# A convolution and two feed-forward layers on one core: the first chunk's tap products are summed by TensorE, its load is split, and the first matmul group starts on parts of its input

## The chip, the cores and the metric

The kernel runs on one core of one Trainium2 chip. The metric is the device time of one execution in microseconds (us), the median of the runs; lower is better.

## The reference

`x` is [2, 4096, 192], `weight_gen` [2, 4096, 8, 7], `w_in` of both layers [192, 2048] and `w_out` [2048, 192], all float32. The reference computes

```
w = exp(wg - max(wg)); w = w / (sum(w) + 1e-9)                 # softmax over the 7 taps
y[b,s,h,g] = sum_k w[b,s,h,k] * x_pad[b, s+k, h, g]            # 6 zero tokens ahead of each sequence
h = y @ w_in1;  g = maximum(0.01*h, h);  y1 = g @ w_out1
h = y1 @ w_in2; r = maximum(h, 0);       out = (r*r) @ w_out2
```

Each of the 192 columns belongs to one of 8 heads of 24; a token's output is the sum of 7 products, each of a window that starts one token later than the last.

## The kernel before

**Chunks and segments.** Partition p holds 64 successive tokens. A chunk is 4 tokens of every partition (512 tokens), and there are 16 chunks. A segment is one layer on one chunk, 32 in all, in the order s = 0, 1 (layer 1 of chunks 0 and 1), then 2 (layer 2 of chunk 0), 3 (layer 1 of chunk 2), and so on in turn. Each float32 operand of a matmul is split into a high part (a copy rounded to fp32r) and a low part (the difference); three products high x high, high x low, low x high make one. The copies and high parts are made by ScalarE (`in_hi` L293, `out_hi` L299, `x_hi` L309 and L312), the low parts by VectorE (`in_lo` L429, `out_lo` L437 and L438, `x_lo` L497 to L502).

**Steps of a segment.** A segment has 8 up steps and 8 down steps. An up step (L700) is 18 matmuls of 512 columns, in 9 pairs, where the two of a pair use the upper and the lower 64 rows of the array, and it fills the two banks of an `h_pair`; there are two such pairs of banks, used in turn. ScalarE then makes `g_hi` (L352) and `g` (L356) of it, VectorE `g_lo` (L569); in layer 2, ScalarE makes `u` (L358), VectorE `g` (L560), ScalarE `g_hi` (L364) and VectorE `g_lo`. A down step (L719, L723) is 20 such matmuls. The order on TensorE is written out in `steps_of`: up 0, up 1, up 2, up 3, down 0, up 4, down 1, up 5, down 2, down 3, up 6, down 4, up 7, down 5, with downs 6 and 7 behind the next segment's ups 0 and 1. Up n waits until `g` of up n-2 has been made (`pair_free`); `g` of n waits for `g_lo` of n-2. In segments 0 and 2 the turn (below) stands between down 4 and up 7.

**The convolution of a chunk** is a list of 19 VectorE operations (`conv_ops`): 6 for the softmax (L450 to L468, with one exp on ScalarE, L303), 7 products of 128x768 (L479) and 6 additions (L484, the last in two halves, L487 and L490). The result is turned by 12 transposes (`turn_x`, L665 and L668) into the h_pair, and `x_hi`, `x_lo`, then `spread_hi` (L320 to L322) and `spread_lo` (L519 to L521) copy it so that each half of the partitions holds what its matmuls need. All of these end before up 0 starts: it waits for both spreads.

**Order of the start.** SP issues, in this order: tap logits of chunk 0 (L208), its window (L198 the 4 tokens of each partition, L203 twice for the 6 tokens of halo), `w_in` piece 0 (L223 and three of L227), `w_out` piece 0 (L237), `w_in` 1, logits and window of chunk 1, `w_out` 1, `w_in` 2, `w_out` 2, `w_in` 3. A layer's weights come in 4 pieces of each kind, in two buffers of each kind, so `w_in` q waits for `in_lo` q-2 and `w_out` q for `out_lo` q-2. VectorE makes chunk 0's convolution with `in_lo` 0, `out_lo` 0 and `in_lo` 1 between its operations, then `x_lo` and `spread_lo`, then two softmax operations of chunk 1. ScalarE makes exp 0, `in_hi` 0, `out_hi` 0, `in_hi` 1, `x_hi`, `spread_hi`. In segment 0 both engines have chunk 1's convolution and the further pieces between the steps (table `IN_FIRST`; pieces at j = 0, 2, 4, 6), in segments 1 and 2 chunk 2's (`IN_SECOND`, `IN_THIRD`) and the pieces of layer 2. Up j with even j in segments 0 and 2 waits for `in_lo` of its piece, and down j for `out_lo`. POOL zeroes the halo of the first rows and makes the identity.

```
conv_ops(0, range(SOFT + 4)); in_lo(0); conv_ops(0, range(SOFT + 4, SOFT + 7)); out_lo(0)
conv_ops(0, range(SOFT + 7, SOFT + 10)); in_lo(1); conv_ops(0, range(SOFT + 10, CONV))
x_lo(0, ...); spread_lo(0, 0); conv_ops(1, (0, 1))            # VectorE ahead of segment 0
```

## Time and profile before

| | us |
|---|---|
| median of 3 runs (lowest to highest) | 1191.36 (1190.73 to 1193.7) |
| the profiled execution | 1191.39 |
| its span, first to last instruction | 1189.6 |
| TensorE matmul busy | 1150.2 (97%) |
| weight loads busy | 1089.3 (92%) |
| VectorE / ScalarE busy | 862.7 (73%) / 668.7 (56%) |

The span leaves about 1.8 us of the profiled execution outside of it. Matmuls overlap in pairs, so the busy time of TensorE says that it is occupied, not that each matmul is as short as it can be; the start-to-start distance of a step says more.

### The profile page before, as it was taken

What the parts mean: (1) busy time and instruction counts of PE and PEld (TensorE: products, weight loads), DVE (VectorE), ACT (ScalarE), POOL (GpSimd) and SP (SyncE); (2) the same over time, 40 slices, a digit from 0 to 9 for tenths busy, and PEclk for the clock granted to TensorE, in tenths of its full rate; (3) what the DMA queues carried; (4) which work ended last, traced back from release to release, by engine and by line L of the source; (5) the groups of instructions that cost most, each with busy time, mean ns of one, the idle gap of its engine ahead of it and who ended that gap; (6) DMA issues with size and microseconds to landing.
All of it is one profiled execution on the core that took longest, in us unless ns stands there. A gap on an engine that the chain in (4) does not pass through costs nothing.

```text
span 1189.6 us, 22593 instructions
## 1 busy us (share of the span) xinstructions
PE 1150.2 (97%) x10112; PEld 1089.3 (92%) x10112; DVE 862.7 (73%) x1048; ACT 668.7 (56%) x817; POOL 3.8 (0%) x11
## 2 busy tenths in 40 slices
PE   0999999999999999999999999999999999999997
PEld 0789899999999999999999999999999999999996
DVE  6778687776778667687776878667687776874664
ACT  2675556646565555555646556565555555556553
POOL 1000000000000000000000000000000000000000
PEclk9999999999999999999999999999999999999999
DMA  8210101000010100101000010100101001000000
GB/s 203 68 54 1 38 15 38 14 27 12 14 38 15 38 1 15 39 15 38 7 17 30 14 38 15 38 1 15 38 14 38 1 15 39 14 1 15 1 1 27
DMA packets 15233, 31.58 MB, mean 27 GB/s; under 512 B 1572, under 2 KB 10914, under 8 KB 15136
## 3 DMA queue, kind: packets, MB, share of 16 engines
q1 hardware_dynamic: 15136, 30.14, 8.1%
q8 instruction: 79, 1.29, 0.5%
q14 instruction: 18, 0.15, 0.0%
HBM read 23.84 MB, written 6.29 MB: 25 GB/s over the span
## 4 chain that ended last, share of the span: by engine, by line
PE 94%; DVE 4%; ACT 1%; DMA 1%; issue 0%; SPq 0%; DVEq 0%; ACTq 0%
PE h_pair L700 44%; PE y_main_psum L719 29%; PE y_rest_psum L723 19%; DVE tap_product L479 1%; DVE conv_out L484 1%; DVE g_lo L569 1%; DMA x_window<-in_x_dram 1%; PE h_pair L665 0%; PE h_pair L679 0%; PE h_pair L682 0%; DVE w_in_parts L429 0%; PE h_pair L668 0%; DVE w_out_parts L438 0%; DVE conv_out L479 0%; DVE w_out_parts L437 0%
## 5 line engine op out<-in xcount | busy, mean ns | idle before, releaser
L700 PE MATMUL h_pair<-x_parts,w_in_parts 64*128 64x512 f32 x4608 | 616.1, 392 | 6.7 <-issue 5.5
L700 PEld LDWEIGHTS h_pair<-x_parts,w_in_parts 64*128 64x128 f32 x4608 | 537.7, 185 | 35.1 <-issue 6.9
L719 PE MATMUL y_main_psum<-g_hi,w_out_parts 64*128 64x512 f32 x2048 | 531.8, 394 | 0.1
L569 DVE TENSOR_TENSOR g_lo<-g,g_hi 128x1024 fp32r<-128x1024 f32 x256 | 313.2, 1223 | 149.7 <-ACT g_hi L364 87.3
L719 PEld LDWEIGHTS y_main_psum<-g_hi,w_out_parts 64*128 64x128 f32 x2048 | 343.6, 185 | 12.2 <-DVE g_lo L569 0.5
L723 PE MATMUL y_rest_psum<-g_lo,w_out_parts 64*128 64x512 f32 x1024 | 297.4, 391 | 0.0
L719 PE MATMUL y_main_psum<-g_lo,w_out_parts 64*128 64x512 f32 x1024 | 297.1, 391 | 0.0
L723 PE MATMUL y_rest_psum<-g_hi,w_out_parts 64*128 64x512 f32 x1024 | 296.7, 391 | 0.0
L352 ACT ACTIVATE g_hi<-h_pair 128x1024 fp32r<-128x1024 f32 x128 | 131.6, 1028 | 197.4 <-PE h_pair L700 197.3
L364 ACT ACTIVATE g_hi<-g 128x1024 fp32r<-128x1024 f32 x128 | 135.8, 1061 | 169.9 <-DVE g L560 169.9
L560 DVE SCALAR_TENSOR_TENSOR g<-h_pair,u 128x1024 f32<-128x1024 f32 x128 | 156.4, 1222 | 72.4 <-ACT u L358 71.7
L723 PEld LDWEIGHTS y_rest_psum<-g_lo,w_out_parts 64*128 64x128 f32 x1024 | 173.7, 185 | 6.1
L723 PEld LDWEIGHTS y_rest_psum<-g_hi,w_out_parts 64*128 64x128 f32 x1024 | 173.9, 185 | 5.5
L719 PEld LDWEIGHTS y_main_psum<-g_lo,w_out_parts 64*128 64x128 f32 x1024 | 173.6, 185 | 5.7
L358 ACT ACTIVATE u<-h_pair 128x1024 f32<-128x1024 f32 x128 | 130.6, 1020 | 79.9 <-PE h_pair L700 78.9
L356 ACT ACTIVATE g<-h_pair 128x1024 f32<-128x1024 f32 x128 | 130.8, 1022 | 1.5 <-DVE g_lo L569 1.5
L479 DVE TENSOR_TENSOR tap_product<-x_window,tap_weights 128x768 f32<-128x768 f32 x96 | 89.9, 952 | 0.0
L484 DVE TENSOR_TENSOR conv_out<-conv_out,tap_product 128x768 f32<-128x768 f32 x80 | 76.2, 953 | 0.5
L531 DVE TENSOR_TENSOR raw_w_in<-y_main_psum,x_window 128x512 f32<-128x512 f32 x16 | 11.1, 692 | 62.5 <-ACT x_window L333 62.5
L333 ACT ACTIVATE x_window<-y_main_psum 128x512 f32<-128x512 f32 x32 | 19.1, 597 | 30.6 <-PE y_rest_psum L723 30.6
L665 PE MATMUL h_pair<-identity,conv_out 64*128 64x64 f32 x128 | 9.8, 228 | 25.2 <-DVE conv_out L490 25.2
L665 PEld LDWEIGHTS h_pair<-identity,conv_out 64*128 64x128 f32 x128 | 9.5, 143 | 26.4 <-issue 23.9
(52 smaller groups left out, 456.8 us busy)
## 6 DMA issues: line engine op xcount, KB each, us to landing
x_window<-in_x_dram SPq DMA_DIRECT2D x14, 960.0 KB, 4.6
out_dram<-raw_w_in SPq DMA_DIRECT2D x16, 384.0 KB, 2.3
raw_w_out<-in_moe_w_out_dram SPq DMA_DIRECT2D x16, 192.0 KB, 3.1
tap_logits<-in_weight_gen_dram SPq DMA_DIRECT2D x16, 112.0 KB, 4.7
raw_w_in<-in_moe_w_in_dram SPq DMA_DIRECT2D x8, 192.0 KB, 3.3
raw_w_in<-in_moe_w_in_dram SPq DMA_DIRECT2D x24, 64.0 KB, 2.8
x_window<-in_x_dram SPq DMA_DIRECT2D x1, 768.0 KB
x_window<-in_x_dram SPq DMA_DIRECT2D x2, 283.5 KB
```

Of the source, the lines that this page charges most:

```text
L352: act.activation(GH[n % 4][:, :, :], hb[pair][:, :, :], ACT.Prelu, alpha=0.01).then_inc(ghi_ready, 1)
L356: act.activation(gate[n % 2][:, :, :], hb[pair][:, :, :], ACT.Prelu, alpha=0.01).then_inc(g_ready, 1)
L358: act.activation(unit[:, :, :], hb[pair][:, :, :], ACT.Relu).then_inc(u_ready, 1)
L364: act.activation(GH[n % 4][:, :, :], gate[n % 2][:, :, :], ACT.Copy).then_inc(ghi_ready, 1)
L479: op = dve.tensor_tensor(dst.rearrange("p (a g) -> p a g", g=G), xwin[slot][:, t * D:(t + TPC) * D].rearrange("p (a g) -> p a g", g=G), ta ...
L484: op = dve.tensor_tensor(total, total, prod[TAP_OPS[i - SOFT][1] % 2][:, :], ALU.add)
L560: dve.scalar_tensor_tensor(gate[n % 2][:, :, :], hb[PAIR[("up", n)]][:, :, :], 0.0, unit[:, :, :], ALU.max, ALU.mult).then_inc(g_ready, 1)
L569: dve.tensor_tensor(GL[n % 4][:, :, :], gate[n % 2][:, :, :], GH[n % 4][:, :, :].bitcast(fp32), ALU.subtract).then_inc(glo_ready, 1)
L665: pe.transpose(h[:, i, t * HP:(t + 1) * HP], conv[r, t, 0:P], ident[r, :])
L700: last = pe.matmul(h[:, i, :], w[r, slot, a, c], v[r, slot, b, :], start=first, stop=end)
L719: return pe.matmul(ym[rows][:, :], w[r, c], g[r, i, :], start=start, stop=stop)
L723: return pe.matmul(yr[rows][:, :], w[r, P:2 * P], g[r, i, :], start=start, stop=stop)
```

## The change

- The window of chunk 0 comes in three parts with a semaphore each: the tokens, the nearer 3 tokens of halo (two transfers), the farther 3 (two transfers). It is the same number of bytes in five transfers where there were three.
- Chunk 0's products are made from tap 6 down to tap 0 and not added on VectorE. Each goes to a buffer of its own (`conv_out`, both `tap_product`, and `g0`, `g1`, `u`, which are idle then; the seventh goes to `conv_out` again), and TensorE turns each with 16 transposes that add to what the banks hold: columns 0 to 127 of a token into h_pair 0, columns 64 to 191 into the two `y_main_psum` banks.
- Ahead of them stand 5 pairs of matmuls of zeroes (`idle`), one pair behind each product and two behind the last. They read `g_hi3`, which POOL zeroes behind the identity, and write the `y_rest_psum` banks.
- Chunk 1 keeps 3 of its 6 additions; its 4 partial sums are turned by 64 transposes (`turn_second`) where 12 stood.
- ScalarE makes `x_hi` of the main part and its spread, then those of the rest, and `in_hi` 1 behind them. VectorE makes `in_lo` 0 behind the products, then `x_lo` and spread in the same two halves, then `in_lo` 1, `out_lo` 0 and chunk 1's two softmax operations.
- The first up is written by itself (`first_up`): each of its 9 pairs waits only for the part that it reads.
- Split pieces move later: on VectorE `in_lo` 2 to segment 0 step 1, `out_lo` 1 to step 2, `in_lo` 3 and `out_lo` 2 to step 4, `out_lo` 3 to step 6; `in_lo` 4, `out_lo` 4, `in_lo` 5, `out_lo` 5, `in_lo` 6 to segment 1 steps 0, 2, 3, 5, 6; `out_lo` 6, `in_lo` 7, `out_lo` 7 to segment 2 steps 0, 2, 3. ScalarE's halves move likewise. SP's order of issue stays, but each piece waits as before for the split two pieces ahead.
- Chunk 2's operations shift by one: segment 2 has six of them where it had five.

The core of the diff (renamed counts and the halves of the split helpers are left out):

```
+    FIRST_OPS = [("times", K - 1 - i, i % (K - 1)) for i in range(K)]
+    SECOND_OPS = []
+    for i in range(K // 2):
+        SECOND_OPS += [("times", K - 1 - 2 * i, i), ("times", K - 2 - 2 * i, K // 2), ("plus", i, K // 2)]
+    SECOND_OPS += [("times", 0, K // 2)]
+    def before(k):
+        return sum([SOFT + len(FIRST_OPS), SOFT + len(SECOND_OPS)][:k]) + max(k - 2, 0) * CONV
...
+        wide = [t[:, :, :].rearrange("p a c -> p (a c)")[:, 0:TPC * D] for t in (gate[0], gate[1], unit)]
+        total = conv[:, :, :].rearrange("p t d -> p (t d)")
+        FIRST = [total, prod[0][:, :], prod[1][:, :]] + wide
+        SECOND = [total, wide[2], prod[1][:, :], prod[0][:, :]]
...
+            def load_first():
+                sync.dma_start(xwin[0][:, HALO * D:WIN],
+                               bass.AP(x_flat.tensor, 0, [[TPP * D, P], [1, TPC * D]])).then_inc(first_loaded[0], 16)
+                half = HALO // 2 * D
                 for start in (0, BOOT):
-                    sync.dma_start(xwin[k][start + 1:start + BOOT, 0:short],
+                    sync.dma_start(xwin[0][start + 1:start + BOOT, half:2 * half],
+                                   bass.AP(x_flat.tensor, (start + 1) * TPP * D - half,
+                                           [[TPP * D, BOOT - 1], [1, half]])).then_inc(near_loaded, 16)
+                for start in (0, BOOT):
+                    sync.dma_start(xwin[0][start + 1:start + BOOT, 0:half],
+                                   bass.AP(x_flat.tensor, (start + 1) * TPP * D - 2 * half,
+                                           [[TPP * D, BOOT - 1], [1, half]])).then_inc(far_loaded, 16)
...
+            pool.memset(GH[3][:, 0, :].bitcast(fp32), 0.0).then_inc(idle_ready, 1)
...
             exp_of(0)
             in_hi(0)
             out_hi(0)
+            x_hi_main(0, PAIR[("first turn",)])
+            spread_hi_main(0)
+            x_hi_rest(0, PAIR[("first turn",)])
+            spread_hi_rest(0)
             in_hi(1)
-            x_hi(0, PAIR[("first turn",)])
-            spread_hi(0)
             for s in range(SEGS):
                 segment(s)
...
+            def first_products(ops):
+                for i in ops:
+                    _, t, b = FIRST_OPS[i]
+                    dve.wait_ge(conv_op, SOFT)
+                    if i == 0:
+                        dve.wait_ge(first_loaded[0], 16)
+                    if i == 1:
+                        dve.wait_ge(near_loaded, 32)
+                        dve.wait_ge(halo_zero, 2)
+                    if t == HALO // 2 - 1:
+                        dve.wait_ge(far_loaded, 32)
+                    if i == K - 1:
+                        dve.wait_ge(product_turned, 1)
+                    times(0, t, FIRST[b]).then_inc(conv_op, 1)
+            def second_sums(ops):
+                for i in ops:
+                    what, t, b = SECOND_OPS[i]
+                    relaxed = what == "times" and 0 < i < len(SECOND_OPS) - 1
+                    dve.wait_ge(conv_op, before(1) + SOFT + (i - 1 if relaxed else i))
+                    if i == 0:
+                        dve.wait_ge(first_loaded[1], 48)
+                        dve.wait_ge(halo_zero, 4)
+                        dve.wait_ge(x_turned, 1)
+                    if what == "times":
+                        op = times(1, t, SECOND[b])
+                    else:
+                        op = dve.tensor_tensor(SECOND[t], SECOND[t], SECOND[b], ALU.add)
+                    op.then_inc(conv_op, 1)
...
-            IN_FIRST = {0: (2, 3, 4, 5, 6), 1: (7, 8), 2: (9, 10), 3: (11, 12), 4: (13, 14), 5: (15, 16), 6: (17, 18)}
-            IN_SECOND = {2: (0, 1), 3: (2, 3, 4, 5), 4: (6, 7), 5: (8, 9), 6: (10, 11), 7: (12, 13)}
-            IN_THIRD = {0: (14,), 2: (15,), 3: (16,), 4: (17,), 5: (18,)}
+            IN_SECOND = {2: (0, 1), 3: (2, 3, 4, 5), 4: (6, 7), 5: (8,), 6: (9, 10), 7: (11, 12)}
+            IN_THIRD = {0: (13,), 2: (14,), 3: (15,), 4: (16,), 5: (17, 18)}
             IN_UP = {0: (0, 1), 2: (2, 3, 4, 5, 6), 3: (7, 8, 9), 4: (10, 11), 5: (12, 13), 6: (14, 15), 7: (16,)}
             IN_DOWN = {0: (17,), 3: (18,)}
+            def first_segment(j):
+                if j == 1:
+                    for i in range(2, SOFT):
+                        softmax(1, i).then_inc(conv_op, 1)
+                    second_sums(range(2))
+                    in_lo(2)
+                if j == 2:
+                    second_sums(range(2, 3))
+                    out_lo(1)
+                    second_sums(range(3, 4))
+                if j == 3:
+                    second_sums(range(4, 6))
+                if j == 4:
+                    in_lo(3)
+                    second_sums(range(6, 7))
+                    out_lo(2)
+                if j == 5:
+                    second_sums(range(7, len(SECOND_OPS)))
+                if j == 6:
+                    out_lo(3)
...
-            conv_ops(0, range(SOFT + 4))
+            for i in range(SOFT):
+                softmax(0, i).then_inc(conv_op, 1)
+            first_products(range(K))
             in_lo(0)
-            conv_ops(0, range(SOFT + 4, SOFT + 7))
+            x_lo_main(0, PAIR[("first turn",)])
+            spread_lo_main(0)
+            x_lo_rest(0, PAIR[("first turn",)])
+            spread_lo_rest(0, (turned_taken, 1))
+            in_lo(1)
             out_lo(0)
-            conv_ops(0, range(SOFT + 7, SOFT + 10))
-            in_lo(1)
-            conv_ops(0, range(SOFT + 10, CONV))
-            x_lo(0, PAIR[("first turn",)])
-            spread_lo(0, 0)
-            conv_ops(1, (0, 1))
+            for i in range(2):
+                softmax(1, i).then_inc(conv_op, 1)
...
+            def idle(pairs):
+                for _ in range(pairs):
+                    for i, r in enumerate(ROWS):
+                        pe.matmul(yr[i][:, :], GH[3][r, 0, 0:P], GH[3][r, 0, :], start=True, stop=True)
+            def turn_product(source, main, rest, apart, first, end):
+                for t in range(TPC):
+                    for c, dst in ((t * D, main), (t * D + HP, rest)):
+                        for i, r in enumerate(ROWS):
+                            last = pe.matmul(dst[i][:, t * HP:(t + 1) * HP], source[r, c:c + P], ident[r, :], is_transpose=True,
+                                             start=first and t == 0 and (apart or dst is main),
+                                             stop=end and t == TPC - 1 and (apart or dst is rest))
+                return last
+            def turn_first():
+                pe.wait_ge(idle_ready, 1)
+                idle(5)
+                main = [hb[0][:, i, 0:QC] for i in range(2)]
+                rest = [ym[i][:, 0:QC] for i in range(2)]
+                for i in range(K):
+                    pe.wait_ge(conv_op, SOFT + i + 1)
+                    done = turn_product(FIRST[FIRST_OPS[i][2]], main, rest, True, i == 0, i == K - 1)
+                    done.then_inc(*((product_turned, 1) if i < K - 1 else (x_turned, 1)))
+                    idle(1 if i < K - 1 else 2)
+            def turn_second(key):
+                pe.wait_ge(conv_op, before(2))
+                pair_free(key)
+                main, rest = ([hb[PAIR[key]][:, i, a:a + QC] for i in range(2)] for a in (0, QC))
+                for b in range(len(SECOND)):
+                    last = turn_product(SECOND[b], main, rest, False, b == 0, b == len(SECOND) - 1)
+                last.then_inc(x_turned, 1)
...
-                    pe.wait_ge(x_hi_spread, s + 1)
-                    pe.wait_ge(x_lo_spread, s + 1)
+                    pe.wait_ge(x_hi_spread, 2 * s + 2)
+                    pe.wait_ge(x_lo_spread, 2 * s + 2)
...
+            def first_up():
+                w, v, h = WI[0], X[0], hb[PAIR[("up", 0)]]
+                def product(slot, a, b, start=False, stop=False):
+                    for i, r in enumerate(ROWS):
+                        last = pe.matmul(h[:, i, :], w[r, slot, a, 0:P], v[r, slot, b, :], start=start, stop=stop)
+                    return last
+                pe.wait_ge(x_hi_done, 1)
+                product(0, 0, 0, start=True)
+                pe.wait_ge(in_lo_done, 1)
+                product(0, 1, 0)
+                pe.wait_ge(x_lo_done, 1)
+                product(0, 0, 1)
+                pe.wait_ge(x_hi_spread, 1)
+                product(1, 0, 0)
+                product(1, 1, 0)
+                pe.wait_ge(x_lo_spread, 1)
+                product(1, 0, 1)
+                pe.wait_ge(x_hi_spread, 2)
+                product(2, 0, 0)
+                product(2, 1, 0)
+                pe.wait_ge(x_lo_spread, 2)
+                product(2, 0, 1, stop=True).then_inc(h_ready, 1)
```

## Rows read from the trace of the kernel before

**Rows 1.** The page: the chain that ended last, by engine.

```profile
PE 94%; DVE 4%; ACT 1%; DMA 1%; issue 0%; SPq 0%; DVEq 0%; ACTq 0%
```

**Rows 2.** The chain in order of time, 0 to 80 us: start, us, engine and line.

```profile
2.09 7.29 DMA x_window<-in_x_dram
...
10.41 1.74 DVE tap_product L479 x2
...
16.49 0.34 DVE w_out_parts L437
16.83 0.60 DVE w_out_parts L438
...
29.16 4.20 PE h_pair L700 x18
...
34.41 0.91 ACT g L356
...
66.28 2.36 PE h_pair L700 x18
...
70.96 2.10 PE h_pair L700 x18
...
75.38 4.19 PE h_pair L700 x36
```

**Rows 3.** The last steps in the same view.

```profile
1181.35 0.26 PE y_rest_psum L723 x2
...
1185.38 0.46 PE h_pair L679 x8
```

**Rows 4.** Timeline, 0 to 61 us: start, us, engine, line, operation [idle before].

```profile
4.27 0.62 POOL L285 TENSOR_SCALAR_AFFINE_SELECT identity<-identity 128x64 f32<-128x64 f32 x2 [0.23 <-POOL identity L282]
...
5.19 0.39 DVE L468 TENSOR_TENSOR tap_weights<-tap_exp,tap_reciprocal 128x224 f32<-128x224 f32 x1
...
13.38 0.84 ACT L299 ACTIVATE w_out_parts<-raw_w_out 128x768 fp32r<-128x768 f32 x1 [1.11 <-DMA raw_w_out<-in_moe_w_out_dram]
...
14.59 1.89 SPq L227 DMA_DIRECT2D raw_w_in<-in_moe_w_in_dram  x3
...
23.98 0.69 PE L665 MATMUL h_pair<-identity,conv_out 64*128 64x64 f32 x8 [23.98 <-DVE conv_out L490]
...
24.43 0.45 PE L668 MATMUL h_pair<-identity,conv_rest 64*128 64x64 f32 x4
...
24.92 0.60 ACT L309 ACTIVATE x_parts<-h_pair 128x512 fp32r<-128x512 f32 x1 [8.55 <-PE h_pair L668]
25.41 0.76 ACT L312 ACTIVATE x_parts<-h_pair 64x256 fp32r<-64x256 f32 x2
26.20 0.69 DVE L497 TENSOR_TENSOR x_parts<-h_pair,x_parts 128x512 fp32r<-128x512 f32 x1 [2.37 <-ACT x_parts L312]
26.20 0.63 ACT L320 ACTIVATE x_parts<-x_parts 64x512 fp32r<-64x512 f32 x1
...
28.64 0.42 DVE L521 CAST x_parts<-x_parts 64x512 fp32r<-64x512 f32 x1
...
38.95 2.36 PE L700 MATMUL h_pair<-x_parts,w_in_parts 64*128 64x512 f32 x18 [1.11 <-ACT g L356]
...
60.40 0.46 PE L665 MATMUL h_pair<-identity,conv_out 64*128 64x64 f32 x8 [1.20 <-DVE conv_out L490]
60.70 0.29 PE L668 MATMUL h_pair<-identity,conv_rest 64*128 64x64 f32 x4
```

**Rows 5.** Stretches: busy us by engine (PE, PEld, DVE, ACT, POOL), granted clock, DMA share, GB/s.

```profile
0.00:5.20 5.20, 0.00 (x0) 0.00 (x0) 1.71 (x6) 1.67 (x2) 3.76 (x11) 1.00 0.53 154
...
102.00:138.00 36.00, 35.60 (x316) 31.97 (x313) 28.29 (x33) 20.02 (x24) 0.00 (x0) 1.00 0.10 31
```

**Rows 6.** Line L227, the loads of `w_in` pieces, 0 to 60 us.

```profile
DMA to landing us min/median/max: 2.6/4.6/7.3
```

**Rows 7.** Timeline of VectorE, segment 2, its seventh up step.

```profile
131.55 1.23 DVE L560 SCALAR_TENSOR_TENSOR g<-h_pair,u 128x1024 f32<-128x1024 f32 x1 [2.24 <-ACT u L358]
```

More of the change, by code:

```diff
@@ L258, in _ @@
             load_in_piece(3)
-            sync.wait_ge(conv_op, CONV)
+            sync.wait_ge(conv_op, before(1))
             load_chunk(2)
@@ L267, in _ @@
                 if c + 3 < NCH:
-                    sync.wait_ge(conv_op, (c + 3) * CONV)
+                    sync.wait_ge(conv_op, before(c + 3))
                     load_chunk(c + 3)
@@ L301, in exp_of, with x_hi_main @@
             def exp_of(k):
-                act.wait_ge(conv_op, k * CONV + EXP + 1)
+                act.wait_ge(conv_op, before(k) + EXP + 1)
                 act.activation(tap_exp[:, :, :], tap_shift[:, :, :], ACT.Exp).then_inc(exp_done, 1)
-            def x_hi(s, pair):
+            def x_hi_main(s, pair):
                 act.wait_ge(x_turned, CHUNK[s] + 1)
@@ L400, in segment @@
                     if NEXT_X[s] is not None and j == (6 if s in LATE_TURNS else 5):
-                        x_hi(s + 1, PAIR[("turn", s)])
-                        spread_hi(s + 1)
+                        x_hi_main(s + 1, PAIR[("turn", s)])
+                        x_hi_rest(s + 1, PAIR[("turn", s)])
+                        spread_hi_main(s + 1)
+                        spread_hi_rest(s + 1)
                     if Y_OUT[s] is not None and j == 5:
@@ L439, in out_lo, with softmax @@
                                   ALU.subtract).then_inc(out_lo_done, 1)
+            def softmax(k, i):
+                slot = 1 if k == 1 else 0
+                if i == 0:
+                    if k < 2:
+                        dve.wait_ge(first_taps_loaded[k], 16)
+                    else:
+                        dve.wait_ge(chunk_loaded, k * 32 - 32)
+                    return dve.tensor_reduce(out=tap_max[:, :], in_=taps[slot][:, :, :], op=ALU.max, axis=AX.X)
+                dve.wait_ge(conv_op, before(k) + i)
+                if i == 1:
+                    return dve.tensor_tensor(tap_shift[:, :, :], taps[slot][:, :, :],
+                                             tap_max[:, :].unsqueeze(2).broadcast_to((P, TH, K)), ALU.subtract)
+                if i == 2:
+                    dve.wait_ge(exp_done, k + 1)
+                    return dve.tensor_reduce(out=tap_sum[:, :], in_=tap_exp[:, :, :], op=ALU.add, axis=AX.X)
+                if i == 3:
+                    return dve.tensor_scalar(tap_den[:, :], tap_sum[:, :], 1e-9, None, ALU.add)
+                if i == 4:
+                    return dve.reciprocal(tap_rec[:, :], tap_den[:, :])
+                return dve.tensor_tensor(tap_w[:, :, :], tap_exp[:, :, :],
+                                         tap_rec[:, :].unsqueeze(2).broadcast_to((P, TH, K)), ALU.mult)
@@ new lines, in times @@
+            def times(k, t, dst):
+                slot = 1 if k == 1 else 0
+                return dve.tensor_tensor(
+                    dst.rearrange("p (a g) -> p a g", g=G),
+                    xwin[slot][:, t * D:(t + TPC) * D].rearrange("p (a g) -> p a g", g=G),
+                    tap_w[:, :, t].unsqueeze(2).broadcast_to((P, TH, G)), ALU.mult)
+            def first_products(ops):
[4 more added lines that the diff above has]
+                        dve.wait_ge(first_loaded[0], 16)
+                    if i == 1:
+                        dve.wait_ge(near_loaded, 32)
[5 more added lines that the diff above has]
+                    times(0, t, FIRST[b]).then_inc(conv_op, 1)
@@ L441, in conv_ops @@
             def conv_ops(k, ops):
[L442 removed]
                 total = conv[:, :, :].rearrange("p t d -> p (t d)")
                 for i in ops:
[L445 to L451 removed]
+                    if i < SOFT:
+                        softmax(k, i).then_inc(conv_op, 1)
@@ L738, in _ @@
             pe.wait_ge(ident_step, 3)
-            turn_x(0, ("first turn",))
+            turn_first()
             for s in range(SEGS):
                 for what, j in steps_of(s):
-                    if what == "up":
+                    if what == "up" and s + j == 0:
+                        first_up()
+                    elif what == "up":
                         up(s, j)
@@ L748, in _ @@
                             down(s, j)
+                    elif s == 0:
+                        turn_second(("turn", s))
                     elif NEXT_X[s] is not None:
```

190 lines of the change are left out of this document (97 added, 93 removed).

## The prediction

> **What bounds the kernel now.** I read the chain of waits first: it runs on TensorE for 94% of the span [rows 1]. From the first up of segment 1 on, the chain in order of time steps by 2.10 us for an up and 2.32 for a down (70.96 to 75.38 less 2.10), back to back [rows 2]; nothing in the change makes these steps fewer or shorter, so what it can win lies ahead of 66.28 us, and the end can only move with them. The same view shows there a wait for the window's load to 9.38, VectorE's products and sums, 12 transposes at 23.98, and the first up at 29.16, 4.20 us long, twice what it takes later [rows 2, 4]. Between 29.16 and 66.28 there are 37.1 us. The work in them is 4.2 + 7 ups of 2.1 + 6 downs of 2.32 + a turn of 0.4 = 33.2, so TensorE lost some 3.9 more, two of its waits being 1.11 at 38.95 (for `g`) and 1.20 at 60.40 (for chunk 1's sums) [rows 4].
>
> **TensorE's clock.** The granted clock reads 1.00 in every stretch of the start, so its level is read from the distances. The first up, with nothing but 12 transposes in 29 us before it, goes at half the later rate (1.2 GHz against 2.4), 0.467 us a pair, and full from 33.36 on. Eight transposes take 0.45 at 23.98 and 0.30 at 60.40, behind full-rate matmuls [rows 4].
>
> **Part by part, until the input is turned.** The tap weights end at 5.58 [rows 4]; the first product (tap 6, tokens alone) may start there. By 5.2 us the DMA engines had moved 154 GB/s x 5.2 = 801 KB [rows 5], which is what logits, tokens and near halo come to (115 + 393 + 290), so the near part lands between 5.2 and 9.38, where the whole window was there. I take 6.9, and 9.5 for the far part. Products go every 0.87 [rows 2]: taps 5 to 3 from 6.9, tap 2 at 9.5, tap 0 from 11.3 to 12.2. Two further transfers on SP, in front of all weight pieces, delay those by 0.7 at most, nothing if the DMA engines stay backlogged.
>
> POOL's identity ends at 4.89. Its memset of 512 columns costs 0.31 (half of the row for two of 64 columns) to 2.5 (eight times that); I take 0.7. Five idle pairs at 0.467 run from 5.6 to 8.0. Then a product's 16 transposes cost 0.90 at the lower level, 0.60 at the full one, and a pair 0.47 or 0.23. The first up went 4.2 us at the lower level before the rise; I take the same stretch here, to 9.8, so products 1 and 2 take 1.37 each and the others 0.83: the last is turned at 14.7. TensorE is the later one here, VectorE 2.5 ahead; `in_lo` 0 hides in that. ScalarE is free at 14.2, when `out_hi` 0 ends (13.38 + 0.84), so neither this nor a load 0.7 later costs more than 0.2.
>
> **To the end of the first up.** ScalarE: main part 14.8 to 15.4, two spreads of 0.63 to 16.6, rests 0.76 to 17.4, spread to 18.1. VectorE: 0.69 from 15.4, two copies of 0.42, then the rests (two of 0.42) from 17.4 and a copy to 18.7. TensorE does its pairs as they come; one is left at 18.7, so `h` of up 0 is ready at 19.0 (33.36 before). If the pairs went at the lower rate, 0.8 later, which the next paragraph absorbs.
>
> **Next late: ScalarE in step 0.** Up 1 runs to 21.1, up 2 to 23.2 (its `in_lo` 1 is done at 19.9). Up 3 waits for `g` of up 1. On ScalarE, behind `g` of up 0 (20.9), stand exp of chunk 1 and `in_hi` 2. The exp waits for VectorE, which makes `in_lo` 1 (19.0 to 19.9), `out_lo` 0 (0.94 [rows 2]) and two softmax operations, until 21.7. `in_hi` 2 waits for its piece: SP's issue ended at 16.48 and L227's transfers took 2.6 to 7.3 [rows 4, 6], 19.1 to 23.8; I take 22.6, near the top, because the transfers ahead of it are the same. Then 0.8, `g_hi` and `g` of 0.91 each plus the last one's tail: 25.4. TensorE stands 2.2 us (1.1 before). `out_lo` 0 now frees its buffer at 20.8, so `w_out` 2 and `w_in` 3 behind it on SP are issued by 24.3 and land by 26.4 to 29; ScalarE asks for `w_in` 3 at 29.5.
>
> **From up 3 to segment 1.** 5 ups, 6 downs and the turn: 10.5 + 13.9 + 64 transposes at 33 to 37.5 ns (12 in 0.40, 8 in 0.30 at 60.40) = 2.2, so 26.6. VectorE's work in segment 0 is 8 `g_lo` of 1.14, ten tap operations of 0.9, softmax 1.4, five splits of 0.9, `x_lo` and copies 2.7: 27, and the sums are done at 42.4, 3 us ahead of the turn. The old wait of 1.20 before the turn goes. After the turn `x_hi`, `x_lo` and copies need about 4.1, beside up 7 and down 5 (4.4). Segment 1 starts at 52.0 instead of 66.28: 14.3 earlier.
>
> **Taken off.** Hand-offs between engines (0.02 to 0.14 each on the chain; some ten to 25.4) add 0.5, at least 0.2 and at most 1.4. In segment 2 VectorE gets `in_lo` 7, `out_lo` 7 beside `out_lo` 6, and a sixth tap operation: 0.87 + 0.94 + 0.9 = 2.7. It was busy 28.3 of 36 us there [rows 5], and had waited 2.24 at 131.55 for `u`, on which up 7 hangs [rows 7]; 2.7 less 2.24 leaves 0.5, between 0 and 2.7. **Sum:** 14.3 - 0.5 - 0.5 = 13.3, rounded down to 13.2. The profiled execution's 1191.39 stands 0.03 above the median, so the forecast is 1178.2.
>
> **Rivals.**
> - The clock does not rise during the turning. What speaks for it: in 4.2 us of the up the array had work all the time; here two thirds of the time are transposes, and no row shows such a mix raising anything. Against: TensorE has full-size matmuls from 5.6 on and is never idle up to 14.7, and the transposes at 1185.38, 3.8 us after the last matmul, still went at the full rate (eight last 0.46 as at 60.40, not 0.69 as at 23.98) [rows 3, 4], so a gap does not drop the clock at once. All seven at 1.37 end at 17.1 instead of 14.7, first up 0.8 slower, up 1 4.2 instead of 2.1; 2.4 + 0.8 + 2.1 less the wait of 2.2 that this fills is 3.1: 1181.3. The Trainium skill, TensorE: Matmul & The Clock Gate, Part 4: PE-mode transpose, says that the full clock does not engage for transposes, as they do not count as TensorE being busy. By that rule this rival is the likelier one; no row here tells it from mine. 15%.
> - VectorE is too full in segment 2 (or 1), and all of the 2.7 stands on the path, as each layer 2 step passes both engines twice: 1180.4. 12%.
> - The split load doesn't do what it says: the near halo lands with the far one at 9.4, since all were issued within 2 us and share the engines. Taps 5 to 0 then end at 14.6, the turning at 15.3 to 15.6, 0.6 to 0.9 later: 1179.0. 7%.
> - **Slower.** A transpose that adds to its bank waits for the one before. Place: 7 x 16 in front of the first up and 64 in the second turn. Before, no transpose adds. The price is from 33 ns, if adding is free, to the 0.20 us that one lasts (0.46 for eight less seven distances) [rows 4]. 176 times the excess over 37.5 ns eats 13.2 us at 0.11 us each; at 0.20 it is 29 us, 1207 with the gain counted. Against it: up matmuls, which do add, follow each other no more slowly than their columns ask. 4%.
>
> **Chances.** Forecast 60%, the rivals 15, 12, 7 and 4, something else 2. The low end: no wait before up 3 (2.2 more), 1176.0. The high end takes in the cold case and a part of the crowding with it: 1182.8. About 0.3% (3.6 us) is what a measurement of this kernel can tell: faster needs less than 1187.8. All but the slower rival and the rest give that: faster 0.93, same 0.03, slower 0.04.
>
> **What would show it.** First product at 5.6 to 5.8 and last at 12.2; last transpose at 14.7; first up's last pair near 19.0 at a distance of 0.23 for the few at its end; up 1 in 2.1 us (4.2: the clock rival); a gap of about 2.2 ahead of up 3, ScalarE's row before it waiting for the load or for the exp; the second turn 2.2 us long without a wait before it; segment 1's first up at 52 to 53; from 100 us on the same distances as before, with segment 3's first up some 0.5 later in its order. The forecast is wrong if transposes lie over 50 ns apart where up matmuls are at full rate, if the near part lands after 9, or if TensorE waits in segments 1 to 3 by more than 1.

## The result, and the profile after

The changed kernel takes 1176.87 us (median of 4 runs, 1175.79 to 1178.2); the kernel before, run beside it, 1191.11 (4 runs, 1190.73 to 1193.7). The ratio is 0.9877, 95% interval 0.9864 to 0.9889: **14.2 us faster**, where 13.2 were forecast. The profiled execution is the shortest of the four, 1175.79 with a span of 1174.0; against the profile of before it gains 15.6. The two gains have to be kept apart below: what follows first is read in the profiled execution.

The page of the changed kernel, busy times and the chain by engine:

```profile
PE 1159.0 (99%) x10290; PEld 1088.7 (93%) x10290; DVE 854.6 (73%) x1036; ACT 668.6 (57%) x816; POOL 4.2 (0%) x12
PE 98%; ACT 1%; DVE 1%; POOL 0%; issue 0%; POOLq 0%; DVEq 0%; ACTq 0%
```

TensorE is on 98% of the chain where it was on 94% [rows 1]; the DMA share is gone. The chain in order of time, changed kernel, 0 to 80 us (start, us, engine and line; up steps are L867, the turn L802):

```profile
5.49 2.50 PE y_rest_psum L795 x10
...
14.14 0.61 ACT x_parts L347
...
20.95 0.39 ACT tap_exp L341
...
22.98 0.92 ACT g L406
23.95 2.35 PE h_pair L867 x18
...
44.20 2.02 PE h_pair L802 x64
...
50.69 2.09 PE h_pair L867 x18
```

This answers to [rows 2]. Three positions are enough to place the gain. Segment 1's first up starts at 50.69 where it started at 66.28: 15.6 earlier, the whole gain of the span. Up 3 of segment 0, the first that waits for anything behind the start, stands at 23.95 where it stood at 38.95 [rows 4]. Segment 3's first up is at 122.26 and was at 138.01 (the row below, of the chain before): 71.57 us after segment 1's where it had been 71.73. Nothing was given back.

```profile
138.01 2.36 PE h_pair L700 x18
```

The timeline of the changed kernel's first 24 us, VectorE, TensorE and ScalarE (start, us, engine, line, operation, the idle time before in brackets):

```profile
5.60 0.96 DVE L524 TENSOR_TENSOR conv_out<-x_window,tap_weights 128x768 f32<-128x768 f32 x1
6.48 1.82 DVE L524 TENSOR_TENSOR tap_product<-x_window,tap_weights 128x768 f32<-128x768 f32 x2
...
10.82 0.95 DVE L524 TENSOR_TENSOR conv_out<-x_window,tap_weights 128x768 f32<-128x768 f32 x1
...
8.58 0.80 PE L795 MATMUL y_rest_psum<-g_hi 64*128 64x512 f32 x2
9.96 0.51 PE L795 MATMUL y_rest_psum<-g_hi 64*128 64x512 f32 x2
...
14.80 2.27 PE L876 MATMUL h_pair<-x_parts,w_in_parts 64*128 64x512 f32 x12 [0.17 <-ACT x_parts L347]
...
23.95 2.35 PE L867 MATMUL h_pair<-x_parts,w_in_parts 64*128 64x512 f32 x18 [0.92 <-ACT g L406]
...
18.57 1.03 ACT L402 ACTIVATE g_hi<-h_pair 128x1024 fp32r<-128x1024 f32 x1 [0.32 <-PE h_pair L876]
20.95 0.39 ACT L341 ACTIVATE tap_exp<-tap_shifted 128x224 f32<-128x224 f32 x1 [0.43 <-DVE tap_shifted L510]
21.24 0.83 ACT L331 ACTIVATE w_in_parts<-raw_w_in 128x768 fp32r<-128x768 f32 x1
```

VectorE's seven products stand back to back from 5.60 to 11.77: no part of the window was waited for, also not the far one, which is read from 9.1 on. The idle pair at 8.58 takes 0.80 and the one at 9.96 takes 0.51: TensorE's clock rose in between, at 10.0, before the first up, whose pairs then go at full rate. `h` of up 0 is there at 18.57 (33.4 before). `in_hi` 2 at 21.24 has no bracket for a load: its piece had landed. TensorE stands 0.92 ahead of up 3, where `g` of up 1 follows that piece on ScalarE.

### The profile page after: what moved, and what is told of

Same layout as the page of the kernel before. It is cut to its first block, busy times and chain, and to the rows that moved or that the text cites. A ratio compares the mean times of both kernels' runs of the same rounds, so it can differ in the third digit from the quotient of the medians.

```text
span 1174.0 us, 22924 instructions
## 1 busy us (share of the span) xinstructions
PE 1159.0 (99%) x10290; PEld 1088.7 (93%) x10290; DVE 854.6 (73%) x1036; ACT 668.6 (57%) x816; POOL 4.2 (0%) x12
## 4 chain that ended last, share of the span: by engine, by line
PE 98%; ACT 1%; DVE 1%; POOL 0%; issue 0%; POOLq 0%; DVEq 0%; ACTq 0%
PE h_pair L867 45%; PE y_main_psum L912 30%; PE y_rest_psum L916 20%; PE y_rest_psum L795 0%; PE h_pair L846 0%; PE h_pair L802 0%; PE h_pair L849 0%; PE h_pair L832 0%; POOL x_window L317 0%; PE h_pair L835 0%; PE y_main_psum L802 0%; ACT w_in_parts L331 0%; DVE g_lo L680 0%; DVE g L671 0%; ACT g_hi L414 0%
## 5 line engine op out<-in xcount | busy, mean ns | idle before, releaser
L867 PE MATMUL h_pair<-x_parts,w_in_parts 64*128 64x512 f32 x4590 | 612.7, 391 | 1.4 <-ACT g L406 0.9
L867 PEld LDWEIGHTS h_pair<-x_parts,w_in_parts 64*128 64x128 f32 x4590 | 531.8, 185 | 32.4 <-ACT g L406 1.4
L524 DVE TENSOR_TENSOR tap_product<-x_window,tap_weights 128x768 f32<-128x768 f32 x91 | 85.2, 950 | 0.0
L580 DVE TENSOR_TENSOR conv_out<-conv_out,tap_product 128x768 f32<-128x768 f32 x70 | 66.5, 950 | 0.5
L383 ACT ACTIVATE x_window<-y_main_psum 128x512 f32<-128x512 f32 x32 | 19.1, 598 | 30.6 <-PE y_rest_psum L916 30.6
L648 DVE TENSOR_TENSOR x_window<-y_rest_psum,x_window 64x512 f32<-64x512 f32 x32 | 22.2, 694 | 1.0
L647 DVE TENSOR_TENSOR x_window<-y_rest_psum,x_window 64x512 f32<-64x512 f32 x32 | 21.9, 683 | 0.4
```

The source lines that it names most:

```text
L524: return dve.tensor_tensor(dst.rearrange("p (a g) -> p a g", g=G), xwin[slot][:, t * D:(t + TPC) * D].rearrange("p (a g) -> p a g", g=G), ...
L580: op = dve.tensor_tensor(total, total, prod[TAP_OPS[i - SOFT][1] % 2][:, :], ALU.add)
L648: dve.tensor_tensor(upper, yr[1][REST:P, :], upper, ALU.add).then_inc(y_free, 1)
L867: last = pe.matmul(h[:, i, :], w[r, slot, a, c], v[r, slot, b, :], start=first, stop=end)
```

## The experiments

Each is the changed kernel with one thing edited. The position of up 3 of segment 0 and of segment 1's first up separate the start from what comes after, since between them TensorE hardly waits, 26.74 us in the changed kernel. Times are of the profiled execution, one for each kernel.

| kernel | `g_hi` of up 0 | up 3 | segment 1 | segment 3 | time |
|---|---|---|---|---|---|
| changed kernel | 18.57 | 23.95 | 50.69 | 122.26 | 1175.79 |
| no idle pairs | 18.79 | 25.36 | 52.11 | 123.86 | 1177.22 |
| idle pairs in front only | 18.02 | 24.87 | 51.60 | 123.17 | 1176.35 |
| window loaded as one | 19.99 | 25.36 | 52.10 | 123.85 | 1177.24 |
| first up waits for all | 22.43 | 27.26 | 53.98 | 125.55 | 1179.07 |
| first sums on VectorE | 23.99 | 29.36 | 56.10 | 127.86 | 1181.28 |
| second sums on VectorE | 18.36 | 23.73 | 49.18 | 121.17 | 1174.61 |
| `in_hi` 2 a step later | 18.79 | 23.42 | 50.25 | 121.83 | 1175.33 |
| and softmax earlier | 17.94 | 22.1 | 48.84 | 120.41 | 1173.8 |
| crowded segment 2 | 18.82 | 24.51 | 51.26 | 124.70 | 1177.96 |

One thing moves in this table that no edit touches. In five of these kernels the same seven products start within 0.1 us of each other, the same idle pairs stand ahead, and `x_hi` waits for nothing but the last transpose. It starts at 13.51 (softmax earlier), 13.93 (second sums on VectorE), 14.14 (changed kernel), 14.36 (`in_hi` 2 later) and 14.77 (first up waits for all), and in the same order the transposes become fast at 8.4, 9.4, 10.0, 10.4 and 11.4. The rows of the first and of the last, with 0.34 for two transposes before and 0.23 to 0.24 behind:

```profile
8.42 0.27 PE L802 MATMUL h_pair<-identity,conv_out 64*128 64x64 f32 x2
```

```profile
11.29 0.30 PE L802 MATMUL y_main_psum<-identity,tap_product 64*128 64x64 f32 x2
```

So the moment at which the clock rises differs by 3 us between runs with the same opening, and it is worth 1.3 us at `x_hi`. A difference below that between two single runs is an edit's only where the rows between say so.

### Is it the idle pairs that raise the clock?

All `idle` calls are taken out:

```
                 pe.wait_ge(idle_ready, 1)
-                idle(5)
...
-                    idle(1 if i < K - 1 else 2)
```

> The changed kernel without any of the idle matmuls. Measure: where the first up of segment 1 starts (50.69 us with the change, 66.28 before) and the rate of up 1. If transposes alone raise TensorE's clock: the turning starts at 6.6, ends by 13.2, up 1 takes 2.1, segment 1 starts at 50.2 to 50.7. If they do not (the clock rival): 16 transposes take 0.86 to 0.9, just about a product's 0.87, so the turning still ends at about 13.2, but up 1 takes 4.2, up 3 starts 1.7 to 2.1 later, segment 1 at 52.4 to 52.8.

Measured 1177.22. Line L802 of this kernel by tile (transposes of the second and third products and of the last but one; count, min, median and max ns of one, stretch), its first up and third wait, and a window over the first up (busy us of PE, PEld, DVE, ACT, POOL, granted clock, DMA share, GB/s):

```profile
L802 PE MATMUL h_pair<-identity,tap_product x16: 311/311/311, 7.6 to 9.1; 64*128 64x64 f32 x16
L802 PE MATMUL y_main_psum<-identity,u x8: 222/224/227, 11.4 to 11.8; 64*128 64x64 f32 x8
...
14.81 3.94 PE L874 MATMUL h_pair<-x_parts,w_in_parts 64*128 64x512 f32 x18 [1.94 <-ACT x_parts L347]
25.36 2.36 PE L865 MATMUL h_pair<-x_parts,w_in_parts 64*128 64x512 f32 x18 [2.13 <-ACT g L406]
14.80:18.60 3.80, 3.79 (x20) 2.60 (x22) 3.02 (x7) 3.37 (x6) 0.00 (x0) 0.55 1.04 292
22.64 0.84 ACT L331 ACTIVATE w_in_parts<-raw_w_in 128x768 fp32r<-128x768 f32 x1 [1.30 <-DMA raw_w_in<-in_moe_w_in_dram]
```

The transposes fell from 311 ns to 224 with nothing but transposes on TensorE: **they raise the clock by themselves**. The rule of the Trainium skill, TensorE: Matmul & The Clock Gate, Part 4: PE-mode transpose, that the full clock does not engage for them, does not hold for these. The rise came at 11.4, as late as in the latest of the runs that have all the pairs. But the granted clock fell at 14.8, at the end of 1.94 us without work, and the first up went at 0.55 in the mean and took 3.94 us instead of some 2.1 plus its short waits. It cost only 0.22 at `h`, because this up's operands come one by one anyway. The other 1.2 us to up 3 is the last row: here `in_hi` 2 waited for its piece until 22.64.

With only the five pairs in front (of the edit above, only its last line):

> The five idle pairs ahead of the turning stay, those between and behind the products go. If the five pairs and the transposes together raise the clock: full rate from about 10, turning ended by 13.4, segment 1 at 50.2 to 50.7. If the pairs between the products are what raises it: up 1 takes 4.2 and segment 1 starts at 52.4 to 52.8.

Measured 1176.35. ScalarE's `x_hi` was held by a late `out_hi` 0 (until 13.6), so TensorE stood 1.61 before the first up, and 2.41 before up 3, where `in_hi` 2 waited for its load until 22.15:

```profile
14.24 2.27 PE L875 MATMUL h_pair<-x_parts,w_in_parts 64*128 64x512 f32 x12 [1.61 <-ACT x_parts L347]
24.87 2.36 PE L866 MATMUL h_pair<-x_parts,w_in_parts 64*128 64x512 f32 x18 [2.41 <-ACT g L406]
```

Both ups go at full rate. So neither set of pairs is needed to raise the clock (it rose at 10.6 here), and without those behind the products `x_hi` came 0.5 earlier. Whether they help to keep it is not shown: it fell without them in one run and not in the other, and below it falls once with more of them.

### What the split load is worth

```
-                    sync.dma_start(xwin[0][start + 1:start + BOOT, half:2 * half], ...).then_inc(near_loaded, 16)
...
+                    sync.dma_start(xwin[0][start + 1:start + BOOT, 0:short], ...).then_inc(first_loaded[0], 16)
...
-                        dve.wait_ge(first_loaded[0], 16)
+                        dve.wait_ge(first_loaded[0], 48)
```

> The window of chunk 0 in three transfers with one semaphore, as before the change; all else as changed. If the split is worth what its place on the chain says: first product at 9.5 instead of 5.60, last at 15.6, last transpose at 16.4 instead of 14.13, up 3 2.2 later, segment 1 at 52.9. If the exp and the w_in piece in front of up 3 hide part of it: at most 1.4 later, 52.1. If the clock falls in the gap behind the idle pairs, up 1 takes 4.2 and it is 54 or more.

Measured 1177.24; the chain and the timeline of this kernel:

```profile
2.08 5.42 DMA x_window<-in_x_dram
...
7.58 0.96 DVE L520 TENSOR_TENSOR conv_out<-x_window,tap_weights 128x768 f32<-128x768 f32 x1 [2.09 <-DMA x_window<-in_x_dram]
...
15.56 0.60 ACT L343 ACTIVATE x_parts<-h_pair 128x512 fp32r<-128x512 f32 x1 [3.44 <-PE y_main_psum L794]
```

The window as a whole was there at 7.50, not at 9.38 as in the run before [rows 2]: the products start 1.98 later, `x_hi` 1.42, segment 1 1.41. So the split gives 1.4 in a run in which the window comes early. Part of that may be the clock, which rose at 12.1 in this run and at 10.0 in the changed kernel. With a window at 9.38 the split would give about 1.9 more, an estimate: no run has the whole load and a late window. That parts do come late at times is in two other runs. VectorE's rows of the kernel without idle pairs, whose first product had started at 5.58, and of the repeat of the changed kernel (below):

```profile
9.40 0.96 DVE L524 TENSOR_TENSOR g<-x_window,tap_weights 128x768 f32<-128x768 f32 x1 [0.26 <-DMA x_window<-in_x_dram]
```

```profile
6.78 1.83 DVE L524 TENSOR_TENSOR tap_product<-x_window,tap_weights 128x768 f32<-128x768 f32 x2 [0.25 <-DMA x_window<-in_x_dram]
```

The far part landed at 9.40 in the one, as late as the whole window before, and cost 0.26; the near part was waited for until 6.78 in the other.

### What the first up by parts is worth

```
-                pe.wait_ge(x_hi_done, 1)
-                product(0, 0, 0, start=True)
+                pe.wait_ge(x_hi_spread, 2)
+                pe.wait_ge(x_lo_spread, 2)
                 pe.wait_ge(in_lo_done, 1)
+                product(0, 0, 0, start=True)
```

> The first up waits for both spreads before its first matmul, as up 0 did before. First up from 18.0 to 20.1 instead of ready at 18.55. If ScalarE's g_hi and g of up 0 are the chain: up 3 some 1.1 later (25.0), segment 1 at 51.7. If the exp (waiting for VectorE until 20.9) and in_hi 2 are the chain: nothing, 50.7.

Measured 1179.07, 3.3 later from up 3 on. Timeline, and the window over the first up:

```profile
18.70 3.69 PE L876 MATMUL h_pair<-x_parts,w_in_parts 64*128 64x512 f32 x18 [3.44 <-ACT x_parts L372]
18.70:22.40 3.70, 3.70 (x20) 3.22 (x22) 2.58 (x5) 0.17 (x1) 0.00 (x0) 0.60 0.45 107
```

The wait of 3.44 was foreseen, its effect on the clock was not: granted 0.60, 3.7 us for the up instead of 2.1. Of the 3.86 at `h`, 0.63 is a later `x_hi` (14.77, the late rise of the clock above), 1.6 the rate, and 1.6 the order. Without the first, which the edit doesn't touch, 2.7 are left of the 3.3. So waiting in small parts does two things, and keeping TensorE supplied is as large as the overlap itself.

### VectorE's sums moved to TensorE, chunk by chunk

Chunk 0 summed on VectorE and turned once, with everything else as changed (loads, order, parts, idle pairs):

```
-    FIRST_OPS = [("times", K - 1 - i, i % (K - 1)) for i in range(K)]
+    FIRST_OPS = [("times", K - 1, 0)]
+    for i in range(K // 2):
+        FIRST_OPS += [("times", K - 2 - 2 * i, 1), ("times", K - 3 - 2 * i, 2), ("plus", 0, 1), ("plus", 0, 2)]
```

> Chunk 0's products are added on VectorE again (6 additions behind the products, 13 operations), and TensorE turns the sum once with 16 transposes; split load, order and idle pairs (one behind each operation) stay. If the additions are worth their place in front of the turning: the last addition ends at about 5.6 + 7 x 0.87 + 6 x 0.93 + 0.4 = 17.7, last transpose at 18.3 instead of 14.13, up 3 4 later, 28.1, segment 1 at about 54.8. If the load of w_in 2 and the exp hide some of it (w_in 2 landed between 21.2 and 22.6 in the runs so far): 1.5 less of it at most.

Measured 1181.28. VectorE's first product and last two sums, an idle pair, the window from 12.8 to 23.0, and the first up:

```profile
6.23 0.96 DVE L526 TENSOR_TENSOR conv_out<-x_window,tap_weights 128x768 f32<-128x768 f32 x1
...
16.41 1.95 DVE L537 TENSOR_TENSOR conv_out<-conv_out,tap_product 128x768 f32<-128x768 f32 x2
...
9.98 0.49 PE L798 MATMUL y_rest_psum<-g_hi 64*128 64x512 f32 x2 [0.34 <-DVE conv_out L537]
12.80:23.00 10.20, 9.23 (x46) 4.72 (x46) 8.65 (x13) 4.15 (x8) 0.00 (x0) 0.50 0.61 179
20.29 3.66 PE L880 MATMUL h_pair<-x_parts,w_in_parts 64*128 64x512 f32 x18
```

Segment 1 starts 5.41 later, all of it from the start: `x_hi` is 5.43 later. Of this 0.63 is not the edit's, since the first product starts at 6.23 here and at 5.60 there, behind a softmax operation that took 0.73 instead of 0.18. The sums end at 18.36; seven products alone ended at 11.77.

The clock did rise: an idle pair takes 0.49 at 9.98 (0.80 at the lower level). But one pair behind each VectorE operation did not hold it. The granted clock is 0.50 from 12.8 to 23.0, although TensorE had not stood idle for more than 0.50 us since 5.5. This costs 0.36 in the turn (eight distances of 0.107 instead of 0.0625) and nothing in the first up: from `x_hi` to `h` are 4.42 us here and 4.43 in the changed kernel. The adding by TensorE is thus the largest single part of the change, about 4.8 of the 15.6.

Chunk 1 the other way, summed whole on VectorE, 16 transposes instead of 64:

```
-    SECOND_OPS = []
+    SECOND_OPS = [("times", K - 1, 0)]
     for i in range(K // 2):
+        SECOND_OPS += [("times", K - 2 - 2 * i, 2), ("times", K - 3 - 2 * i, 3), ("plus", 0, 2), ("plus", 0, 3)]
```

> Chunk 1's products are all added on VectorE (3 more additions, in segment 0) and turned by 16 transposes instead of 64. If VectorE had slack there: the turn takes 0.5 instead of 2.02, with no wait before it, and segment 1 starts 1.5 earlier than with the change for the same start of up 3 (26.7 us after it with the change, 25.2 here). If VectorE is too full: a wait ahead of the turn of up to 2.9 that eats the gain, or glo late for a down.

Measured 1174.61, segment 1's first up 25.45 after up 3 instead of 26.74:

```profile
43.97 0.50 PE h_pair L801 x16
...
49.18 2.36 PE h_pair L865 x18
```

The turn is 0.50 instead of 2.02 and waits for nothing: VectorE has the time for the three additions. **This part of the change costs 1.3 us** at segment 1 (1.52 less a short wait ahead of it), and 0.9 by segment 3's first up, which is 97.44 after up 3 here and 98.31 in the changed kernel; where the 0.4 between are lost stays open. It moves work from an engine with slack to the one that bounds. The slack is used up by it, though: in the changed kernel VectorE stands idle 1.10 at 43.88 and 2.40 at 47.51, and here it has no idle time from 18.1 to 49.1.

### ScalarE in step 0

`in_hi` 2, which both the load and VectorE's exp operand can hold, goes behind the next `g`:

```
                             exp_of(1)
-                            in_hi(2)
                         if j == 1:
+                            in_hi(2)
                             out_hi(1)
```

> ScalarE makes in_hi of w_in piece 2 behind g of step 1 instead of ahead of g_hi of step 1. If in_hi 2 and its load are what up 3 waits for: up 3 starts at 23.2 (the exp still waits for VectorE until 20.95) whatever the load does, segment 1 at 49.9 to 50.0. If something behind it takes over (in_lo 2 late for up 4, as it is needed at 27): no gain.

Measured 1175.33: the wait before up 3 fell from 0.92 to 0.2, segment 1 to 50.25. What was left was the exp's wait for VectorE; so chunk 1's two softmax operations go ahead of `in_lo` 1 and `out_lo` 0 as well:

```
+            for i in range(2):
+                softmax(1, i).then_inc(conv_op, 1)
             in_lo(1)
             out_lo(0)
-            for i in range(2):
-                softmax(1, i).then_inc(conv_op, 1)
```

> As e7, and VectorE makes chunk 1's first two softmax operations ahead of in_lo 1 and out_lo 0, so that the exp does not wait. Up 3 starts right behind up 2, at 22.8, segment 1 at 49.5. Rival: in_lo 1, 0.8 later, holds up 2 (needed at 20.7, made by 20.0), or w_in 3, issued 0.8 later, holds in_hi 3 and g_hi of step 3: then 50 or more.

Measured 1173.8. ScalarE and TensorE of this kernel:

```profile
19.77 0.39 ACT L341 ACTIVATE tap_exp<-tap_shifted 128x224 f32<-128x224 f32 x1
20.04 1.03 ACT L402 ACTIVATE g_hi<-h_pair 128x1024 fp32r<-128x1024 f32 x1
...
17.73 6.74 PE L867 MATMUL h_pair<-x_parts,w_in_parts 64*128 64x512 f32 x54
```

54 matmuls in one row: ups 1, 2 and 3 without a wait, and segment 1 at 48.84. Behind the exp stands `g_hi` of up 1, where `in_hi` 2 stood. Of the 1.85 gained, 0.63 is an earlier `x_hi` (13.51, the early rise of the clock above), which the edit doesn't touch.

### The two together, timed beside the changed kernel

The first has both edits, chunk 1 summed on VectorE, and idle pairs in front and behind only (`idle(0 if i < K - 1 else 3)`).

> e8's order, e6's sums of chunk 1 on VectorE, and the idle pairs between the products taken out (five ahead and three behind stay). If the three act on different stretches of the path: up 3 at 22.0 as in e8, segment 1 at 47.5 (25.4 behind it, as in e6), 3.2 before the changed kernel's 50.69: 1172.6 in time where the changed kernel has 1175.8, and about 4 under its median. Rival: with VectorE's additions ahead of it the sums are late for the turn, or the load of w_in 3 holds step 3: no better than e8.

> e8 again, timed. If the load of w_in 2 is what spreads the changed kernel's runs (1175.8 to 1178.2): median 2 to 3 below the changed kernel's, about 1174, and the runs closer together. If up 3's wait was the whole of it: 1.2 to 1.9 below.

> The changed kernel once more, timed beside e9 and e10: median 1176 to 1177.5. Its in_hi 2 starts between 21.2 and 22.7, and up 3 and segment 1 move with it: up 3 at 2.7 behind the start of in_hi 2, segment 1 26.7 behind up 3.

| kernel | median us of 4 runs | lowest to highest | ratio to before, 95% |
|---|---|---|---|
| changed kernel again | 1176.2 | 1176.0 to 1178.28 | 0.9879, 0.9865 to 0.9894 |
| step 0 early | 1174.92 | 1174.54 to 1175.15 | 0.9864, 0.985 to 0.9879 |
| all three | 1174.05 | 1173.68 to 1174.43 | 0.9856, 0.984 to 0.9873 |

No run of one lies within the runs of another, though the intervals overlap. The last is 2.1 below the changed kernel and 17.0 below the one before (1191.1). The parts would promise 2.6 (1.3 by the medians for step 0, 1.3 for chunk 1). Segment 1 was expected at 47.5 and came at 49.06: its turn waited 0.2 and its first up 0.86, put down to no releaser. TensorE, and below it VectorE's `x_lo` and the last of its three copies:

```profile
43.03 0.71 PE h_pair L801 x16
...
48.20 0.86 issue
49.06 2.36 PE h_pair L865 x18
```

```profile
46.21 0.69 DVE L592 TENSOR_TENSOR x_parts<-h_pair,x_parts 128x512 fp32r<-128x512 f32 x1
...
48.54 0.42 DVE L630 CAST x_parts<-x_parts 64x512 fp32r<-64x512 f32 x1
```

`x_hi` had ended at 44.4, but `x_lo` stands behind `out_lo` 3 and a `g_lo` on VectorE and starts at 46.21, with no idle time before it; the last copy ends at 48.96, 0.10 before the up. VectorE has no idle time at all from 16.7 on. With the sums alone moved, the same copy ended at 49.08 and the up started at 49.18. So with chunk 1's additions on it VectorE bounds segment 0, an earlier TensorE has to wait for it there, and the two savings don't add up in full.

The repeat of the changed kernel also shows where its spread of 2.4 can come from. Its profiled execution is the longest of the four, 1178.28 (timeline of ScalarE and TensorE, and windows over the start of up 3 and over what follows):

```profile
22.25 0.84 ACT L331 ACTIVATE w_in_parts<-raw_w_in 128x768 fp32r<-128x768 f32 x1 [0.71 <-DMA raw_w_in<-in_moe_w_in_dram]
...
24.97 3.87 PE L867 MATMUL h_pair<-x_parts,w_in_parts 64*128 64x512 f32 x18 [1.75 <-ACT g L406]
24.90:25.40 0.50, 0.43 (x4) 0.38 (x6) 0.50 (x2) 0.50 (x2) 0.00 (x0) 1.00 1.05 205
25.00:29.00 4.00, 4.00 (x22) 3.12 (x24) 4.00 (x6) 3.33 (x5) 0.00 (x0) 0.57 0.86 290
```

`w_in` 2 landed a microsecond later and was waited for 0.71, up 3 waited 1.75 instead of 0.92, and 0.4 behind the start of up 3 the clock fell: 3.87 us for an up of 2.35. Segment 1 is at 53.27, 2.6 late: 1.0 up to the start of up 3 (0.7 the load, 0.2 a later `x_hi`) and 1.6 from the rate. The other long executions, 1177.43 and 1178.2 in the first four, have no trace. Their mean granted clock is 0.997, as in this one, and 0.998 to 0.999 in the short ones; that points the same way and does not prove it, since another kernel reads 0.997 at 1175.33. The kernel with step 0 early, which has no such wait, spreads by 0.6.

### Is there slack left in segment 2?

Three reductions over 128x768 are put on VectorE in segment 2's steps 2 to 4; their results are not used.

```
+                        if j in (2, 3, 4):
+                            dve.tensor_reduce(out=spare[j - 2][:, :], in_=xwin[0][:, 0:TPC * D]..., op=ALU.max, axis=AX.X)
```

> The changed kernel with three further VectorE reductions of 128x768 (some 0.8 each) in segment 2, steps 2 to 4; they are of no use to the result. Measure: segment 3's first up less segment 1's, 71.57 with the change and 71.73 before. If the change has used up all the slack (no wait ahead of g of step 6 now): 73.6 to 74.0. If there is slack left: under 72.

Measured 1177.96. First VectorE's `g` in step 6 of segment 2 and the window over that segment in the changed kernel (VectorE is the third busy time), then TensorE's up 7 and segment 3's first up in the crowded one:

```profile
115.89 1.22 DVE L671 SCALAR_TENSOR_TENSOR g<-h_pair,u 128x1024 f32<-128x1024 f32 x1
86.00:122.00 36.00, 35.85 (x318) 28.70 (x314) 30.86 (x37) 20.42 (x25) 0.00 (x0) 1.00 0.10 31
```

```profile
119.59 2.36 PE L871 MATMUL h_pair<-x_parts,w_in_parts 64*128 64x512 f32 x18 [1.30 <-DVE g L672]
...
124.70 2.35 PE h_pair L871 x18
```

Segment 3 comes 73.44 after segment 1, against 71.57: of 2.6 added, 1.87 is lost, 1.30 of it before one up that waits for `g`. In the changed kernel `g` of step 6 stands without the idle time of 2.24 that it had [rows 7], and VectorE is busy 30.86 of 36 us where it was 28.29 [rows 5]. So the change used the slack up to its last 0.7 us, and paid nothing.

## Why the prediction was right

It was right in direction, place and size: the gain lies ahead of segment 1 and nowhere else, and 1176.87 is 1.3 below the forecast, in the range. Step by step:

- **Start of the turning.** First product 5.60 (5.58). The near part was there by 6.48, so the assumed wait until 6.9 did not exist; the last product ended at 11.77, 0.4 early. The idle pairs began at 5.49 and the clock rose at 10.0 (9.8 said). That this came so close is in part luck: with the same opening it rose between 8.4 and 11.4 in other runs. Last transpose 14.13 (14.7). A product and its idle pair took 1.39 at the lower level and 0.78 at the full one (1.37 and 0.83 said).
- **First up.** `x_hi` at 14.14 (14.8), `h` at 18.57 (19.0). The eight short steps between engines were laid out right, in one order.
- **Up 3.** This is the one term that was mis-sized: 23.95 against 25.4. I had `w_in` 2 at 22.6, from the upper half of 19.1 to 23.8. It was there by 21.24 in the profiled run, and at 22.15, 22.25 and 22.64 in three others. With 22.64 in the run without idle pairs up 3 stood at 25.36, as worked out; so the sum was right for a late load, and the load varies. The exp's wait for VectorE (21.7 said, 20.95 measured) was the second holder, as named.
- **From up 3 to segment 1.** 26.74 (26.6); the turn 2.02 (2.2), `x_hi` and the spreads hidden, as said. The wait of 1.20 went.
- **Taken off.** 0.5 for hand-offs and 0.5 for segment 2 were both too much: the listed times already hold them, and segment 2's give-back was 0. These two and the load are the whole 2.4 by which the profiled execution is better than the forecast; the median is better by 1.3.

Of the rivals, **the clock that doesn't rise** is out: it rose in every run in which the products were turned one by one, and with transposes alone too. But one argument against it was weak: from the last turn, 3.8 us after the last matmul [rows 3], I took that a gap does not drop the clock at once. In later runs it fell during a gap of 3.44 us, at the end of one of 1.94, 0.4 us behind one of 1.75, and once with no gap over 0.50; it stayed up over gaps of 0.92, 1.24, 1.61, 2.13 and 2.41. The length of the last gap doesn't decide, and what does stays open. **Crowding in segment 2** was near: the next 2.6 us cost 1.9. **The split load that does nothing** is out: in the profiled run its parts came before they were asked for, and with the far part as late as 9.40 it was still waited for by only 0.26. **Transposes that wait for the one before** is out: 64, nearly all adding, in 2.02 us, 31.6 ns each, no dearer than the 33 to 37.5 of those that don't add [rows 4].

What I did not ask is whether chunk 1's partial sums are worth their turn. The text counted 1.20 of wait gained and 1.8 of transposes paid in the same sum, and took the total; VectorE being 3 us ahead of the turn, as it said, meant that three additions of 0.87 were free.

Undone one by one, the adding for chunk 0 (4.8), the parts of the first up (2.7) and the split load (1.4), less the loss at chunk 1 (1.3), make 7.6 of the 15.6 at segment 1. Each is read from one run, cleared of what its rows show to be no part of the edit. For the rest no run was made. By the rows it is work that no longer stands ahead of `x_hi` (`out_lo` 0, `in_lo` 0 and 1 on VectorE, some 0.9 each), the clock that rises before the first up and not in it (2.1, in part counted with its parts), the window, which came by 9.1 at the latest and perhaps at 7.50 as in the run that loads it as one, where it had been 9.38, and that is no merit of the change, and the wait of 1.20 before the second turn.

## What to carry over

A sum may go to the matrix engine while that engine waits for it, and should stay off it where the vector engine is ahead: the same edit gave 4.8 us for chunk 0 and cost 0.9 to 1.3 for chunk 1. Before two savings are added, ask which engine bounds once the first is made: here VectorE took over and kept a part of the second. Let the first matmuls wait for parts of their input, since a whole wait of 3.4 us cost 1.6 for the order and 1.6 for the rate of the up behind it. On an engine that works in order, put nothing that waits for a load in front of what the bounding engine waits for: it makes the time worse and, by four runs of each, its spread too (2.4 us against 0.6).

## What was not expected of the hardware

Transposes of 64x64 raised TensorE's clock with no other matmul on it, from 311 to 224 ns each. With the same opening the rise came between 8.4 and 11.4 us. The clock fell by gaps of 1.75 and 1.94 us and stayed up over 2.13 and 2.41, and it fell once where TensorE was never idle for more than 0.50 at a time; an up at the lower level takes 3.7 to 3.9 us instead of 2.1 to 2.4. The window of chunk 0 landed at 7.50 in the run that loads it as one and at 9.38 in the kernel before, with the same transfers, and the far part of it at 9.40 in a third run; `w_in` 2 landed by 21.24 in one and at 22.64 in another, with the same transfers ahead of it.
